# Heads 0 and 1 of a fused attention kernel prepared and searched in another order; in every slot ScalarE copies a head's scores before it makes the threshold difference of an earlier head

## The reference

```python
scores = scale * np.matmul(q, k.transpose(0, 1, 3, 2))      # 2 batches, 8 heads, 576 x 576, head_dim 64
kth = np.partition(scores, -32, axis=-1)[..., -32:-31]
scores = np.where(scores >= kth, scores, -1000000000.0)
attn = softmax(scores)
x = np.matmul(attn, v)                                       # -> (1152, 512)
# x -> top-1 mixture of 8 experts (1024 wide) -> rational-function MLP (2048 wide)
```

## Time and profile before

| | |
|---|---|
| median of 3 runs | 801.8 us (801.5 to 803.18) |
| the profiled execution, its own time | 802.91 us |
| its span, first to last instruction | 801.2 us |
| busy share of the span | PE 93%, DVE 82%, ACT 61%, POOL 45% |
| attention (the 72 units) | about the first 343 us |
| share of the chain that ended last | PE 58%, DVE 25%, DMA 5% |

### The profile page before, as it was taken

The page is one execution under the profiler, slowest core; times in us unless marked ns, Lnnn a source line. Parts: engine busy times, 40 slices in busy tenths (PEclk is TensorE's granted clock), DMA queues, the critical chain, the costliest instruction groups (busy, mean ns, idle before and its releaser), DMA issues.

```text
span 801.2 us, 15628 instructions
## 1 busy us (share of the span) xinstructions
PE 747.6 (93%) x5417; PEld 697.3 (87%) x5417; DVE 657.6 (82%) x1664; ACT 491.5 (61%) x890; POOL 359.7 (45%) x531
## 2 busy tenths in 40 slices
PE   5899999999999999837999999999899999999997
PEld 4788899898888888737999999999879988989996
DVE  3999999999999999825667667666659998898885
ACT  6677676666677876433454445444547877677673
POOL 4646565545468784240000000000049868767764
PEclk8799999999999999967999999999999999999999
DMA  9740000600000203022567685776911002000001
GB/s 193 172 151 14 1 16 1 224 15 2 14 2 15 107 2 106 1 121 57 211 167 234 179 258 189 214 188 187 269 41 40 0 1 80 1 1 27 13 1 39
DMA packets 61978, 71.20 MB, mean 89 GB/s; under 512 B 21969, under 2 KB 41937, under 8 KB 61906
## 3 DMA queue, kind: packets, MB, share of 16 engines
q1 hardware_dynamic: 60466, 65.57, 28.2%
q0 software_dynamic: 1440, 4.72, 1.7%
HBM read 56.12 MB, written 14.16 MB: 88 GB/s over the span
## 4 chain that ended last, share of the span: by engine, by line
PE 58%; DVE 25%; issue 5%; DMA 5%; ACT 3%; POOL 2%; SPq 1%; DVEq 0%; ACTq 0%; POOLq 0%
PE bank L1416 16%; PE bank L1417 15%; PE bank L1418 15%; DVE best L750 8%; DVE pairs L752 6%; PE bank L1317 3%; DVE best L771 3%; DVE pairs L733 3%; DVE pairs L769 3%; PE bank L1293 2%; PE bank L1283 2%; DMA slots_out<-y_blocks 2%; DMA slot_rows<-slots_in 2%; DVE joined L780 1%; PE bank L1269 1%
## 5 line engine op out<-in xcount | busy, mean ns | idle before, releaser
L968 DVE RECIPROCAL r<-c 128x384 f32<-128x384 f32 x48 | 122.5, 2551 | 20.7 <-POOL c L689 19.9
L1039 ACT ACTIVATE probsT<-bank 96x768 f32<-96x768 f32 x72 | 58.2, 808 | 95.5 <-PE bank L1300 95.5
L750 DVE MAX8 best<-pairs 128x8 f32<-128x288 f32 x288 | 115.7, 443 | 0.0
L678 POOL DMA_INDIRECT x_rows<-slots_out,slot_index x9 | 11.2, 1239 | 225.8 <-DMA slots_out<-y_blocks 224.3
L1317 PE MATMUL bank<-v_rows,probsT 96*128 96x65 f32 (+1 forms) x960 | 106.6, 264 | 3.6 <-ACT probsT L1039 3.4
L1317 PEld LDWEIGHTS bank<-v_rows,probsT 96*128 96x128 f32 (+1 forms) x960 | 102.5, 181 | 8.0 <-ACT probsT L1039 6.6
L897 DVE TENSOR_TENSOR wl<-raw,wh 128x1024 fp32r<-128x1024 f32 x72 | 87.1, 1216 | 19.2 <-ACT wh L1133 18.9
L752 DVE MATCH_REPLACE8 pairs<-best,pairs 128x288 f32<-128x288 f32 x216 | 94.5, 442 | 0.0
L1147 ACT ACTIVATE hTh<-bank 128x288 fp32r<-128x288 f32 x64 | 26.4, 413 | 103.4 <-PE bank L1418 103.4
L1416 PE MATMUL bank<-xTh,wh 128*128 128x288 f32 x256 | 76.7, 299 | 13.0 <-DVE xTl L909 13.0
L588 POOL TENSOR_TENSOR pairs<-scores 128x288 int32<-128x288 int32 x72 | 57.6, 800 | 66.4 <-ACT scores L1025 66.1
(11 more groups left out here) (140 smaller groups left out, 2155.1 us busy)
## 6 DMA issues: line engine op xcount, KB each, us to landing
raw<-in_moe_w SPq DMA_DIRECT2D x16, 2048.0 KB, 9.1
slots_in<-zeros SPq DMA_DIRECT2D x18, 256.0 KB
slot_rows<-slots_in SPq DMA_DIRECT2D x32, 144.0 KB, 8.8
slots_out<-y_blocks SPq DMA_DIRECT2D x32, 144.0 KB, 8.1
raw<-in_moe_w_in SPq DMA_DIRECT2D x8, 512.0 KB, 8.0
v_rows<-in_v SPq DMA_DIRECT2D x16, 144.0 KB, 5.0
out_rows<-out_rows SPq DMA_DIRECT2D x9, 256.0 KB, 2.3
q_rows<-in_q SPq DMA_DIRECT2D x8, 256.0 KB, 2.9
```

What stands on the lines that cost most here:

```text
L750: ins = nc.vector.max(best, cur)
L968: nc.vector.reciprocal(rS[x][:], cS[x][:]).then_inc(s_d2, 1)
L1039: nc.scalar.activation(pT[x % 2][:], T_ps[0:KP, 0:KJ * P], ACT.Exp, scale=SCALE).then_inc(s_ex, 1)
```

## The change

The start of all four instruction streams is in another order, and `scores_out` and `short_of` have changed places in all slots of ACT.

- ACT rounds keys 2 and 3 directly after it has copied out key 0, ahead of `q_out(0, 1, 0)`, on which `scores(0)` waits.
- The second half of tile 0's queries and key 3 (to be turned and copied) move into slots 0 and 1: slot i (0 to 4) now prepares key 3+i, where slot i (0 to 3) prepared key 4+i, and slots 0 and 1 also take `q(0, 0, 1)` and `q(0, 1, 1)`.
- DVE does M1, R1 and L1 of unit 0 before `greater(1)`.
- POOL fills its constants first, makes both low parts together, and makes unit 1's sum last.
- PE turns key 2 before `scores(1)`.

```diff
-        FIRST_K, FIRST_Q = 4, 2
+        FIRST_K, FIRST_Q = 3, 2
@@ q_pieces
+            if i in (0, 1):
+                return [(0, i, 1)]
@@ USE
         for what in (("k", 0, 0), ("k", 0, 1), ("q", 0, 0, 0), ("q", 0, 1, 0), ("k", 1, 0), ("k", 1, 1),
-                     ("k", 2, 0), ("k", 2, 1), ("q", 0, 0, 1), ("q", 0, 1, 1), ("k", 3, 0), ("k", 3, 1)):
+                     ("k", 2, 0), ("k", 2, 1)):
@@ gpsimd
-            for g in (2, 3):
-                k_low(g)
-                sum_pairs(g - 2)
-            less_greater(0)
             nc.gpsimd.memset(vn[:, :, :, D:DV], 1.0).then_inc(s_vo, 1)
             nc.gpsimd.memset(zeros[:], 0.0).then_inc(s_zm, 1)
+            k_low(2)
             k_low(FIRST_K)
+            sum_pairs(0)
+            less_greater(0)
+            sum_pairs(1)
@@ vector
             greater(0)
+            of_greater(0, M1)
+            of_greater(0, R1)
+            of_lesser(0, L1)
             greater(1)
@@ scalar, slot
+                if i + 2 < NH:
+                    scores_out(i + 2)
                 if 0 <= i - 2 < NH:
                     short_of(i - 2)
-                if i + 2 < NH:
-                    scores_out(i + 2)
@@ scalar, start
             k_out(0, 0)
             k_out(0, 1)
+            k_high(2)
+            k_high(FIRST_K)
             q_out(0, 1, 0)
             k_out(1, 0)
             k_out(1, 1)
-            k_high(2)
             scores_out(0)
-            k_high(3)
-            scores_out(1)
             k_out(2, 0)
             k_out(2, 1)
-            q_out(0, 0, 1)
-            q_out(0, 1, 1)
-            k_high(FIRST_K)
-            k_out(3, 0)
-            k_out(3, 1)
+            scores_out(1)
@@ tensor, start
             scores(0)
-            scores(1)
             k_turn(2, 0)
             k_turn(2, 1)
-            q_turn(0, 0, 1)
-            q_turn(0, 1, 1)
-            k_turn(3, 0)
-            k_turn(3, 1)
+            scores(1)
```

More of the change, by code:

```diff
@@ L394, in fused @@
         M1, R1, M2, R2, M3, R3, M4, L1, LR, L2, JOIN, FIN = range(12)
-        TK = {}
+        TK = {(0, M1): 1, (0, R1): 2, (0, L1): 3}
         for i in range(NH + 1):
@@ L398, in fused @@
                           (i - 1, JOIN), (i, L2), (i - 1, FIN)):
-                if 0 <= x < NH:
+                if 0 <= x < NH and (x, st) not in TK:
                     TK[x, st] = len(TK) + 1
@@ L799, in _ @@
                 n, h = divmod(i, H)
-                of_greater(i, M1)
+                if i:
+                    of_greater(i, M1)
                 of_greater(i - 1, M3)
@@ L803, in _ @@
                     sums(n - 1)
-                of_greater(i, R1)
+                if i:
+                    of_greater(i, R1)
                 of_greater(i - 1, R3)
-                of_lesser(i, L1)
+                if i:
+                    of_lesser(i, L1)
                 of_greater(i, M2)
```

## The result

The changed kernel took 804.76 us (median of 10 runs, 803.88 to 805.82), the kernel before 801.65 (10 runs, 800.05 to 803.77): ratio 1.0037, 95% interval 1.0024 to 1.0049, which is 3.0 us slower (1.9 to 3.9). The forecast was 803.9 against 801.8, +2.1, in a range of 800.6 to 805.8. In a later set of runs the same two kernels gave 1.0040 (1.0025 to 1.0054), so +3 us stands.

The account below looks back on a forecast made before the run. Attention was taken to run at DVE's pace, 4.42 us a slot, with PE and ACT holding DVE at the start. A start 3.0 us later less 0.9 from the swap gave +2.1: 803.9 against 801.8, range 800.6 to 805.8.

Parts of the forecast that it names:

- Step 1: At the start, ACT waits for keys 2 and 3 until 10.04 us, so `scores(0)` begins at 12.20 instead of 9.65.
- Step 2: Units 0 to 2: at half clock each further unit adds 2.50 us, putting `greater(2)` at 19.10, where it was 18.97.
- Step 3: Slots 0 and 1: query copies moved there on ACT make `scores(4)` begin at 26.57, 2.5 us late.
- Step 4: Slots from unit 4 to 7: PE is behind, at half clock for the first slot; `greater(7)` at 44.8, 3.0 us late.
- Step 5: All ACT slots: scores copied ahead of `short_of` shorten DVE's three waits after 94 us, gaining 0.9 us.
- Clock back at 28.9: PE's full clock returns as before, at about 28.9 us: +0.7, 802.5; chance 0.30 together with an earlier key landing.
- Full clock throughout: PE keeps full clock through the start, and the change gains: -1.8 us, 800.0; chance 0.12.
- Late `short_of`: In tiles 1 to 8 `short_of` comes too late for the drop: up to 2 us on top, 806; chance 0.08.
- Keys landing sooner: ACT's wait at the key DMA is shorter: 802.9 with 1 us less; counted within a shared chance of 0.30.

Follow-up runs that it names:

- The DMA of their own: The changed kernel, but keys 2 and 3 have a DMA and a semaphore of their own, ahead of keys 4 to 7: ratio 0.9995 to the kernel before.
- The early search steps: The kernel before, with M1, R1 and L1 of unit 0 ahead of `greater(1)` and unit 0's difference ahead of unit 1's sum on POOL: ratio 0.9995.
- the filler: The changed kernel with 26 added matmuls of 512 columns in PE's pauses, into PSUM that nobody reads: ratio 1.0006 to the kernel before.

## Why the prediction was right, point by point

**Step 1** (ACT stands at the key DMA) holds. `scores(0)` was forecast at 12.20 and began at 12.40; the keys landed 8.5 us after their issue rather than 8.3. The DMA of their own shows that it is this wait, and what it costs: 2.3 us at every later event for 2.16 us less of standing.

**Step 2** (three units on the path, half clock) holds in kind: `greater(2)` 19.69, forecast 19.10. Each unit took 2.7 or 2.6 instead of 2.50, since from a unit's start on PE to ACT's copy it was 1.31 to 1.34 at half clock from a standing start, not 1.22. That steps 1 and 2 would cancel within 0.2 us is therefore 0.7. The early search steps were forecast to be worth nothing, and alone they are.

**Step 3** (query copies in slots 0 and 1) holds: `scores(4)` 27.13 against 26.57 forecast, waiting for `qT_low`, and the experiment that moves them back takes 1.9 us off that start.

**Step 4** (PE behind, at half clock) holds with a term too small. Forecast were 5.28 us for the slot from unit 4 to unit 5; it took 6.02. Of this 0.53 is a wait for ACT's copy of key 4 (`kT`), which the forecast had only in the slots after it. Half clock lasted to 32.9 and not only to the end of the forecast slot at 31.85. From there the forecast fits: 5.40 and 5.38 for the next two slots (5.39), 2.18 from the last scores to `greater` (2.17). `greater(7)` was forecast at 44.8 and is at 46.11, a cost of 4.3 instead of 3.0: 0.6 of the difference from step 2, 0.7 from this slot. That the clock makes much of this is shown by the filler; how much differs from execution to execution.

One sentence of step 4 was wrong. I read the clock as 1.00 for the first matmuls. The query turns at 6.50 and 7.35 us took 1.06 us each, as they do at half clock (the one at 13.76 in the earlier trace rows), and 0.60 at full: PE started at half clock, and the column shows 1.00 only where no record exists yet.

```profile
6.50 1.06 PE L1256 MATMUL bank<-ident,q_rows_high 128*64 128x128 f32 x4
...
38.20 0.60 PE L1256 MATMUL bank<-ident,q_rows_high 128*64 128x128 f32 x4 [0.78 <-ACT kT L991]
```

So this trace does agree with the Trainium skill ("TensorE: Matmul & The Clock Gate", "What's actually happening") that the throttled state is the default. No term of the sum rested on it.

**Step 5** (the swap) had the right sign, but the 0.9 was counted on the wrong waits. I took the three waits of the earlier trace rows for the kernel's own; 1.4 of the 1.6 us came with a stretch of half clock that the profiled execution of before happened to have. Behind unit 7 the swap gives 0.3 us where that stretch is absent, as in the profile after, and 1.0 where it is present. In the runs it is worth 2.0 in the new start and 1.1 in the old one, more than the profiles show, and that rest stays open. The cover of 0.2 us for the drop sufficed: neither PE's waits nor DVE's show `short_of`.

**The sum.** The cost of the start was forecast too small (3.0, measured 4.3), and what comes back later too (0.9; 1.9 to unit 71 in these profiles, of which 0.3 is the swap and 1.6 the stretch, and 0.7 behind it). The errors have opposite signs. That +2.1 came near +3.0 is in part luck; the mechanism of the start, on which the sign hangs, was right.

**The rivals.** Clock back at 28.9: not in this profile. Full clock throughout: only with filler, and then the changed kernel is about as fast as before (1.0006), not 1.8 us faster as I had reckoned. Late `short_of`: did not occur. Keys landing sooner: not in this profile (8.5 us), but made so by the DMA of their own. From `greater(71)` to the end of the span the profile after took 474.2 us and that of before 474.9. The 13 profiles lie between 474.2 and 475.4 there; the cause was not looked for, and the forecast had taken these layers for a block that only moves.

## To carry to other kernels

Before an instruction is moved forward on an in-order queue, look up when its data land: what was ready by luck at the old place is a wait at the new one, and everything behind it inherits the wait. Taking work out of the prologue into the loop pays only if the loop's engines have room there; here ACT and PE had none in the first slots. Of two copies of which one feeds the engine that sets the pace, that one goes first: here this was worth 1.1 us in the old start, and more where a stretch of half clock had used up the slack. Before a wait in a profile is counted as something to be won, look whether it is there in a second execution.

## What the runs showed of the hardware

- Executions of one kernel differ by where PE's clock falls, on a single core. The kernel before has two groups, 803.7 us (mean clock 0.972 to 0.974) and 801.3 (0.976 and above), and their medians come again on the two other chips (803.6 and 801.5; 803.5 and 801.5). The profiled one of before was at half clock from 94 to 97 us in the middle of dense work:

```profile
94.00:97.00 3.00, 3.00 (x14) 2.63 (x14) 3.00 (x12) 0.92 (x2) 1.74 (x2) 0.50 0.00 0
```

- In these profiles this stretch comes at one place of the program or not at all. Ahead of it PE waits 0.59 us for a copy (`kT`) and makes eight small matmuls for the gate (1.03 us); the clock falls 1.3 to 1.5 us behind these, while PE works on without a pause. So it was in 3 of 13 profiles (from 93.9, 95.1 and 102.2 us); in the other ten the same place ran at full clock.
- A late start can cost more than its own lateness through this: the changed kernel's slot of unit 5 took 5.40 us in one execution and 8.62 in another.
- A row's granted clock of 1.00 is no evidence at the start of a trace; the duration of a known matmul is. In the changed kernel's second profile the column shows 1.00 from 33 to 40 us, where the matmuls took 0.44 us instead of 0.30; its first lower value is at 102 us. For the same reason a run's mean clock can come out too high: this longest of the runs has 0.981.
